# Growth factors as constants, opening loads and operand sums in another order, first batch's queries decayed by VectorE, in a fused retention and two-layer feed-forward kernel

## The chip, the cores and the metric

The kernel runs on one core of one Trainium2 chip. The metric is the device time of one execution in microseconds (us). Three runs of the kernel before took 589.05, 589.28 and 590.81 us; the median is 589.28 us.

## The reference

```python
# attention: q, k, v are (2 batches, 8 heads, 768, 64)
gamma = 1.0 - 2.0 ** (-5.0 - np.arange(H))
for t in range(S):
    state = gamma * state + outer(k[:, :, t], v[:, :, t])
    y[:, :, t] = scale * q[:, :, t] @ state
# x: 1536 tokens of 512
h = x @ w_in                      # 512 -> 2048
x = (h * sigmoid(1.702 * h)) @ w_out
xn = x / rms(x) * rms_g
x = (silu(xn @ w_gate) * (xn @ w_val)) @ w_out   # 512 -> 1536 -> 512
```

## The kernel before

Attention is done in 12 steps `a`: six chunks of 128 tokens for each of two batches, all eight heads in one step. A step has four kinds of products on TensorE: `scores` (L374, k by q, inside the chunk), `from_state` (L406, the decayed queries by the running state; the first chunk of a batch has none), `new_products` (L391, decayed k by v, summed in PSUM; the last chunk has none) and `from_chunk` (L419, masked scores by v). VectorE multiplies the scores by a mask (`masked`, L874) and scales the running sum into a state (`new_state`, L886 and L889). GpSimd multiplies k by a decay table (`decay_k`, L1008) and q by another (`decay_q`, L1016). ScalarE copies the result out (`copy_y`, L671). Steps go in pairs: scores of both, then the rest.

The running sum is never rescaled, so `decay_k` of chunk c needs a table that has grown by gamma to the power of -128 c. These tables are made at the start: two rows of the first table are loaded and broadcast by two small transfers, VectorE multiplies them, GpSimd takes the power -1 (L1037), VectorE refines it (L859 to L863) and multiplies tables 1 to 4 (L867, L870). Every step counts up the semaphore `decay_set`, and `masked(0)` and the first `decay_q` wait for its last value (GpSimd's wait stands after `decay_k(0)`).

Inputs come into four slots of 2048 columns, each in two transfers of 512 KB: q and k features first (`load`, semaphore `qk_in`), k and v tokens first (`load_kv`, `kv_in`). Two queues issue them, SyncE's and ScalarE's. In the trace SyncE issues, in this order, q/k of slots 0 and 1 (at 0.7 and 1.2 us), the mask (1.6), k/v of slot 2 (2.1), q/k of slots 2 and 3 (2.8 and 3.5), k/v of slot 3 (4.2) and the first weights (4.8); ScalarE issues the two rows (0.7 and 1.2), the decay table of 6 KB (1.6), k/v of slots 0 and 1 (2.1 and 2.9) and the query table (3.6). Later loads wait until a slot is free: `load(b)` for the scores and the decayed queries of step b - 4, `load_kv(b)` for its `y_done`.

The feed-forward layers use Strassen-like products: a hidden unit has seven products M1 to M7 of half-size blocks, each six matmuls of 384 columns (L457, L459, L460), from operands split into a high and a low part. Seven operands are made of x: B11, B21 and B22 are plain blocks of x; T1 to T4 are sums (`sum_x`, on VectorE; T1 and T3 together, then T2 from T3, then T4 from T2). ScalarE makes the high part (`split_x`, L599), VectorE the low (`lower_x`, L758); the weights go through `weight_sum` on GpSimd (four sums), `split_w` on ScalarE (L580) and `lower_w` on VectorE (L749). Semaphores count, so a product waits for the place of its operand in a fixed order: `UPPER` gives that of the high parts, and the low parts of the first phase go by the operand's own number. For the first phase this is woven into the attention steps of both engines by `if a == ...`; the rest comes at the start of the first hidden unit, n = 0. A hidden unit writes three PSUM banks. ScalarE copies M1 into the bank of M6 (`copy_m1`, L632), M5 into SBUF (`copy_m5`, L638), and the bank of M6 into SBUF (`copy_u2`, L644), which must be done before M7 adds to that bank.

All engines run their own program in order; nothing but the semaphores links them.

## Time and profile before

| | |
|---|---|
| median of three runs | 589.28 us (589.05 to 590.81) |
| the profiled execution's own time | 590.75 us |
| span of the profile | 588.96 us, shown as 589.0 |
| busy TensorE / VectorE / ScalarE / GpSimd | 576.1 / 354.0 / 298.2 / 175.7 us |
| DMA | 52.85 MB, mean 90 GB/s |

The profiled execution took 1.79 us more than its span, for what lies around it. A busy number counts the time in which an engine has an instruction in work; what limits the kernel is read from the idle stretches of TensorE and from its clock, which is granted at one of two levels, 1.2 GHz (0.50 in the windows view) or 2.4 GHz (1.00). The view has no record of the clock ahead of 10.17 us and shows 1.00 there; the matmuls' durations tell which level it was.

### The profile page before, as it was taken

To read this page: it belongs to the slowest core of one execution; us is meant where nothing else is said; L and a number is where in the kernel's file an instruction comes from. 1 tells how busy PE (TensorE), PEld (TensorE's weight loads), DVE (VectorE), ACT (ScalarE), POOL (GpSimd) and SP (SyncE) were. 2 spreads that over 40 slices of the span, in tenths; PEclk is the share of its full clock that TensorE was granted. 3 is DMA by queue.
4 is the path that set the end of the run, shared out by engine and by line. 5 is a ranking of instruction groups with operands and counts; after the bars stand their busy time and mean duration, and the time that the engine had idled before them with its cause. 6 is when DMAs were issued, how large, how long until landed. Compare 5 with 4: busy or idle time off the path is not lost.

```text
span 589.0 us, 9342 instructions
## 1 busy us (share of the span) xinstructions
PE 576.1 (98%) x3638; PEld 554.5 (94%) x3638; DVE 354.0 (60%) x459; ACT 298.2 (51%) x501; POOL 175.7 (30%) x189
## 2 busy tenths in 40 slices
PE   6899999999999999999999999999999999999997
PEld 6788999999999999999999999998889999998886
DVE  2379555566444665876435778668763666667332
ACT  1134666754334776645327655564534555554321
POOL 2758344100040544000223464420050545430000
PEclk9699999999999999999999999999999999999999
DMA  8892222322211222322112222223212422223202
GB/s 292 279 332 90 71 73 72 102 77 72 73 36 37 71 73 73 105 74 72 37 36 73 72 72 72 73 72 108 63 46 76 140 72 72 71 73 108 71 1 107
DMA packets 24652, 52.85 MB, mean 90 GB/s; under 512 B 2208, under 2 KB 2336, under 8 KB 24608
## 3 DMA queue, kind: packets, MB, share of 16 engines
q1 hardware_dynamic: 23744, 50.93, 28.4%
q10 hardware_dynamic: 864, 1.33, 0.6%
q8 instruction: 29, 0.48, 0.3%
q14 instruction: 15, 0.12, 0.1%
HBM read 49.10 MB, written 3.15 MB: 89 GB/s over the span
## 4 chain that ended last, share of the span: by engine, by line
PE 92%; issue 3%; DVE 2%; POOL 1%; DMA 1%; ACTq 0%; POOLq 0%; DVEq 0%
PE bank L507 20%; PE twin L507 20%; PE twin L457 11%; PE twin L460 10%; PE twin L459 10%; PE bank L460 6%; PE bank L457 6%; PE bank L459 6%; DMA arena<-tables 1%; PE bank L406 1%; PE bank L419 1%; PE bank L391 1%; PE twin L374 1%; DVE x_lo L758 1%; POOL arena L1016 1%
## 5 line engine op out<-in xcount | busy, mean ns | idle before, releaser
L749 DVE TENSOR_TENSOR w_lo<-raw,w_hi 128x512 fp32r<-128x512 f32 (+2 forms) x148 | 148.8, 1021 | 50.6 <-ACT w_hi L580 50.4
L1023 POOL TENSOR_TENSOR raw<-raw 128x256 f32<-128x256 f32 x40 | 30.6, 765 | 319.9 <-DMA raw<-w 319.9
L457 PE MATMUL twin<-x_hi,w_hi 128*128 128x384 f32 x360 | 120.6, 335 | 0.9 <-DVE w_lo L749 0.9
L460 PE MATMUL twin<-x_hi,w_lo 128*128 128x384 f32 x360 | 120.4, 334 | 0.0
L459 PE MATMUL twin<-x_lo,w_hi 128*128 128x384 f32 x360 | 120.3, 334 | 0.0
L580 ACT ACTIVATE w_hi<-raw 128x512 fp32r<-128x512 f32 (+2 forms) x148 | 109.0, 763 | 19.2 <-PE bank L507 7.6
L784 DVE TENSOR_TENSOR g_lo<-arena,g_hi 128x768 fp32r<-128x768 f32 x56 | 54.8, 979 | 75.9 <-ACT g_hi L610 75.9
L610 ACT ACTIVATE g_hi<-arena 128x768 fp32r<-128x768 f32 x56 | 47.5, 848 | 103.5 <-PE bank L507 103.5
L457 PEld LDWEIGHTS twin<-x_hi,w_hi 128*128 128x128 f32 x360 | 67.6, 188 | 1.2 <-DVE w_lo L749 1.2
L459 PEld LDWEIGHTS twin<-x_lo,w_hi 128*128 128x128 f32 x360 | 67.6, 188 | 0.0
L460 PEld LDWEIGHTS twin<-x_hi,w_lo 128*128 128x128 f32 x360 | 67.6, 188 | 0.0
L459 PE MATMUL bank<-x_lo,w_hi 128*128 128x384 f32 x200 | 66.9, 334 | 0.0
L457 PE MATMUL bank<-x_hi,w_hi 128*128 128x384 f32 x200 | 66.9, 334 | 0.0
L460 PE MATMUL bank<-x_hi,w_lo 128*128 128x384 f32 x200 | 66.9, 334 | 0.0
L1033 POOL TENSOR_TENSOR raw<-raw 128x256 f32<-128x256 f32 x40 | 45.1, 1128 | 0.0
L507 PE MATMUL twin<-g_lo,w_hi 128*128 128x384 f32 x128 | 42.8, 334 | 0.0
L507 PE MATMUL twin<-g_hi,w_lo 128*128 128x384 f32 x128 | 42.8, 334 | 0.0
L507 PE MATMUL bank<-g_hi,w_hi 128*128 128x384 f32 x128 | 42.8, 334 | 0.0
L507 PE MATMUL twin<-g_hi,w_hi 128*128 128x384 f32 x128 | 42.8, 334 | 0.0
L507 PE MATMUL bank<-g_hi,w_lo 128*128 128x384 f32 x128 | 42.8, 334 | 0.0
L507 PE MATMUL bank<-g_lo,w_hi 128*128 128x384 f32 x128 | 42.8, 334 | 0.0
L1029 POOL TENSOR_TENSOR raw<-raw 128x256 f32<-128x256 f32 x40 | 39.3, 981 | 3.1
(107 smaller groups left out, 1002.8 us busy)
## 6 DMA issues: line engine op xcount, KB each, us to landing
raw<-w SPq DMA_DIRECT2D x68, 512.0 KB, 3.7
arena<-attn_in SPq DMA_DIRECT2D x22, 512.0 KB, 6.5
out<-x SPq DMA_DIRECT2D x1, 1536.0 KB, 8.6
out<-x SPq DMA_DIRECT2D x6, 256.0 KB, 2.0
arena<-attn_in ACTq DMA_DIRECT2D x2, 512.0 KB, 10.7
arena<-tables SPq DMA_DIRECT2D x1, 512.0 KB, 7.5
arena<-tables ACTq DMA_DIRECT2D x1, 256.0 KB, 12.8
ident<-ident_in SPq DMA_DIRECT2D x1, 64.0 KB, 13.4
```

The source lines that it names most:

```text
L374: mm = pe.matmul(acc[2 * par + h][:, cols(p, P)], k[rows, cols(p, P)], q[rows, cols(p, P)], start=True, stop=True)
L457: pe.matmul(dst, w_hi[q][:, w], x_hi[:, x], start=start and kk == 0, stop=False, skip_group_check=True)
L459: pe.matmul(dst, w_hi[q][:, w], x_lo[:, x], start=False, stop=False, skip_group_check=True)
L460: mm = pe.matmul(dst, w_lo[q][:, w], x_hi[:, x], start=False, stop=kk == 1, skip_group_check=True)
L507: mm = pe.matmul(dst, a, x, start=f == 0 and k == 0, stop=f == TILES[layer] - 1 and k == 2, skip_group_check=True)
L580: act.activation(w_hi[q % 3][:, dst], src, ACT.Copy).then_inc(w_hi_done, 1)
L610: act.activation(g_hi[ft % 3][:, :], g32[:, cols(f, SEQ)], ACT.Copy).then_inc(g_hi_done, 1)
L749: dve.tensor_tensor(w_lo[q % 3][:, dst], src, w_hi[q % 3][:, dst].bitcast(F32), ALU.subtract)\
L784: dve.tensor_tensor(g_lo[ft % 3][:, :], g32[:, cols(f, SEQ)], g_hi[ft % 3][:, :].bitcast(F32), ALU.subtract).then_inc(g_lo_done, 1)
L1023: pool.tensor_tensor(s1, a21, a22, ALU.add).then_inc(w_sums, 1)
L1029: pool.tensor_tensor(s4, a12, s2, ALU.subtract).then_inc(w_sums, 1)
L1033: pool.tensor_tensor(a21, a11, a21, ALU.subtract).then_inc(w_sums, 1)
```

## The change

- The growth factors of chunks 1 to 4 are constants: 16 memsets of one column on VectorE and 16 on GpSimd, then one product of 32 columns on VectorE for all four tables. The two row loads, the power and its refinement are gone. `masked(0)` waits for `decay_set` 4, `decay_k(1)` for 1.
- Opening loads: q/k of slot 1 and k/v of slot 2 go to ScalarE's queue, k/v of slot 1 to SyncE's. ScalarE's order is decay table, k/v 0, q/k 1, query table, k/v 2; SyncE's is q/k 0, mask, k/v 1, q/k 2, q/k 3, k/v 3, weights.
- TensorE does `new_products(0)` between `scores(0)` and `scores(1)`.
- `decay_q` of steps 1 to 5 is VectorE's; GpSimd keeps steps 7 to 11. Each batch has its own semaphore.
- In the first phase the plain blocks are split first and T2, T3 and T4 later; in unit n = 0 T4 is summed and split after `copy_m5`, and the products come in the order M1, M5, M2, M3, M6, M7 instead of M1, M5, M6, M2, M3, M7. GpSimd waits for six low parts (`x_lo_done`) before the weight sums of the second unit.

```diff
-UPPER = {True: (B11, B21, T3, T1, B22, T2, T4), False: (B11, B21, T1, T2, B22, T3, T4)}
+UPPER = {True: (B11, B21, B22, T1, T3, T2, T4), False: (B11, B21, T1, T2, B22, T3, T4)}
+LOWER = {True: (B11, B21, T1, B22, T2, T3, T4), False: (B11, B21, T1, T2, B22, T3, T4)}
...
+        def growth(c, h):
+            return (1.0 - 2.0 ** (-5.0 - h)) ** (-CHUNK * c)
...
             load(0)
-            load(1)
             sp.dma_start(table[:, T_MASK:T_Q], tables[:, T_MASK:T_Q]).then_inc(mask_in, 16)
-            load_kv(2)
+            load_kv(1)
...
                 scores(a)
+                if a == 0:
+                    new_products(0)
                 scores(a + 1)
                 if a == 0:
-                    new_products(0)
                     from_state(0)
...
-            for k, row in enumerate((first_row, next_row)):
-
-                at_ = (CHUNK - 2) * k
-                act.dma_start(row, tables[at_:at_ + 1, T_K:T_K + HEADS].to_broadcast([P, HEADS])).then_inc(rows_in, 16)
             act.dma_start(table[:, 0:T_MASK], tables[:, 0:T_MASK]).then_inc(decay_in, 16)
-            for a in range(2):
-                act.dma_start(slot[a][:, 1024:2048], attn_in[BATCH * a, :, 1024:2048]).then_inc(kv_in[a], 16)
+            act.dma_start(slot[0][:, 1024:2048], attn_in[0, :, 1024:2048]).then_inc(kv_in[0], 16)
+            act.dma_start(slot[1][:, 0:1024], attn_in[BATCH, :, 0:1024]).then_inc(qk_in[1], 16)
             act.dma_start(table[:, T_Q:T_ALL], tables[:, T_Q:T_ALL]).then_inc(q_table_in, 16)
+            act.dma_start(slot[2][:, 1024:2048], attn_in[2 * BATCH, :, 1024:2048]).then_inc(kv_in[2], 16)
...
-            dve.wait_ge(rows_in, 32)
-            dve.tensor_tensor(growth, first_row, next_row, ALU.mult).then_inc(decay_set, 1)
...
+            for c in range(1, 3):
+                for h in range(HEADS):
+                    ins = dve.memset(factor(c, h), growth(c, h))
+            ins.then_inc(factors_set, 1)
+            dve.wait_ge(factors_set, 2)
             dve.wait_ge(decay_in, 16)
...
                 masked(a)
                 if a == 0:
                     new_state(0)
+                    decay_q(1)
                 masked(a + 1)
-                if a == 4:
+                if a < 4:
+                    decay_q(a + 2)
+                elif a == 4:
                     lower_x(0, B11)
...
                     if n > 0:
                         lower_w(r, 1)
                     else:
+                        sum_x(0, T4)
                         lower_x(0, T4)
...
+                    if n == 0:
+                        split_x(0, T4)
                     split_next(r, 0)
                     copy_u2(n)
...
                 if kind == "hidden":
+                    if r == 1:
+
+                        pool.wait_ge(x_lo_done, 6)
                     for k in range(4):
```

How the instructions move, at three places. First ScalarE's queue at the start of the program, before (L659 the rows, L660 the decay table, L662 k/v of slots 0 and 1, L663 the query table):

```order
L659 DMA arena<-tables 128x8 x2
L660 DMA arena<-tables 128x12
L662 DMA arena<-attn_in 128x1024 x2
L663 DMA arena<-tables 128x512
L665 ACT_TABLE_LOAD
```

and now (L673 the decay table, L674 k/v of slot 0, L675 q/k of slot 1, L676 the query table, L677 k/v of slot 2):

```order
L673 DMA arena<-tables 128x12
L674 DMA arena<-attn_in 128x1024
L675 DMA arena<-attn_in 128x1024
L676 DMA arena<-tables 128x512
L677 DMA arena<-attn_in 128x1024
```

The decay table and k/v of slot 0 stand first; the query table still has two loads of 512 KB ahead of it.

VectorE's first two pairs of steps, before (L874 `masked`, L886 and L889 `new_state`):

```order
L874 TENSOR_TENSOR arena<-twin,arena 128x1024 [waits scores_done,decay_set,mask_in]
L886 COPY arena<-bank 128x256 [waits kv_done]
L874 TENSOR_TENSOR arena<-twin,arena 128x1024 [waits scores_done]
L889 TENSOR_TENSOR arena<-bank,arena 128x256 [waits kv_done]
L889 TENSOR_TENSOR arena<-bank,arena 128x256 [waits cross_done,kv_done]
```

and now (L884 `masked`, L896 and L899 `new_state`, L910 `decay_q`):

```order
L884 TENSOR_TENSOR arena<-twin,arena 128x1024 [waits scores_done,decay_set,mask_in]
L896 COPY arena<-bank 128x256 [waits kv_done]
L910 TENSOR_TENSOR arena<-arena 128x512 [waits qk_in1,q_table_in]
L884 TENSOR_TENSOR arena<-twin,arena 128x1024 [waits scores_done]
L910 TENSOR_TENSOR arena<-arena 128x512 [waits qk_in2]
L899 TENSOR_TENSOR arena<-bank,arena 128x256 [waits kv_done]
L910 TENSOR_TENSOR arena<-arena 128x512 [waits cross_done,qk_in3]
L899 TENSOR_TENSOR arena<-bank,arena 128x256 [waits cross_done,kv_done]
```

The second mask now stands behind a `decay_q` that waits for the query table, and two more stand between the masks and the states.

ScalarE around the start of the first hidden unit, before (L599 `split_x`, L671 `copy_y`, L632 `copy_m1`, L638 `copy_m5`, L580 `split_w`, L644 `copy_u2`):

```order
L599 ACTIVATE x_hi<-x_0 128x768 [waits x_sums]
L671 ACTIVATE x_1<-bank 128x2x2x128 [waits y_done] x2
L599 ACTIVATE x_hi<-x_0 128x768 [waits x_sums]
L632 ACTIVATE twin<-twin 128x384 [waits probs_done,m1_done]
L638 ACTIVATE arena<-twin 128x384 [waits m5_done]
L580 ACTIVATE w_hi<-raw 128x768 [waits w_sums]
L644 ACTIVATE arena<-twin 128x384 [waits m6_done]
```

and now (L616, L685, L649, L655, L597, L661 in the same roles):

```order
L616 ACTIVATE x_hi<-x_0 128x768 [waits x_sums]
L685 ACTIVATE x_1<-bank 128x2x2x128 [waits y_done] x2
L649 ACTIVATE twin<-twin 128x384 [waits probs_done,m1_done]
L655 ACTIVATE arena<-twin 128x384 [waits m5_done]
L616 ACTIVATE x_hi<-x_0 128x768 [waits x_sums]
L597 ACTIVATE w_hi<-raw 128x768 [waits w_sums]
L661 ACTIVATE arena<-twin 128x384 [waits m6_done]
```

The split of T4, with its wait for VectorE's sum, has gone from ahead of `copy_m1` to between `copy_m5` and `copy_u2`.

## Rows read from the trace of the kernel before

**Rows 1.** Stretches: us, busy us (instructions) of each engine, TensorE clock, DMA share, GB/s.
```profile
13.59:23.83 10.24, 8.19 (x95) 7.34 (x92) 2.39 (x4) 1.19 (x2) 6.71 (x6) 0.50 0.91 330
23.83:57.00 33.17, 31.24 (x572) 28.89 (x570) 26.77 (x29) 11.43 (x18) 24.75 (x20) 1.00 0.65 223
77.00:575.00 498.00, 498.00 (x2764) 482.80 (x2763) 306.39 (x397) 268.97 (x452) 132.82 (x146) 1.00 0.25 71
```

**Rows 2.** Waits of TensorE over the whole span: us in total, times, longest.
```profile
PE bank L391 <- POOL arena L1008: 3.4, 2, 2.9
PE bank L406 <- POOL arena L1016: 2.8, 2, 2.0
```

**Rows 3.** Issues from 0.5, 1.5, 2.0 and 3.6 us on: count, KB, us to landing.
```profile
arena<-attn_in SPq DMA_DIRECT2D x1, 512.0 KB, 5.7
...
arena<-tables SPq DMA_DIRECT2D x1, 512.0 KB, 7.5
arena<-tables ACTq DMA_DIRECT2D x1, 6.0 KB, 7.7
...
arena<-attn_in SPq DMA_DIRECT2D x1, 512.0 KB, 9.6
arena<-attn_in ACTq DMA_DIRECT2D x1, 512.0 KB, 9.7
...
arena<-tables ACTq DMA_DIRECT2D x1, 256.0 KB, 12.8
```

**Rows 4.** Timeline, opening: start, us, engine, line, tiles, count [idle before <- releaser].
```profile
6.48 3.79 PE L374 MATMUL twin<-arena 64*128 64x128 f32 x32 [0.80 <-DMA arena<-attn_in]
...
12.01 1.04 POOL L1008 TENSOR_TENSOR arena<-arena 128x512 f32<-128x512 f32 x1 [2.12 <-DVE arena L870]
...
12.05 1.23 DVE L874 TENSOR_TENSOR arena<-twin,arena 128x1024 f32<-128x1024 f32 x1
...
13.76 1.98 PE L419 MATMUL bank<-arena 128*64 128x128 f32 x16
...
16.47 1.26 POOL L1016 TENSOR_TENSOR arena<-arena 128x512 f32<-128x512 f32 x1 [3.42 <-DMA arena<-tables]
...
17.79 1.97 PE L406 MATMUL bank<-arena 64*64 64x128 f32 x16 [2.05 <-POOL arena L1016]
...
19.69 1.12 PE L391 MATMUL bank<-arena 128*64 128x64 f32 x16
...
23.30 2.29 PE L374 MATMUL twin<-arena 64*128 64x128 f32 x32
```

**Rows 5.** Timeline, chunks 6 to 9, TensorE at its upper level.
```profile
37.20 2.06 PE L374 MATMUL twin<-arena 64*128 64x128 f32 x32
...
41.55 1.92 PE L419 MATMUL bank<-arena 128*64 128x128 f32 x32
...
45.84 1.97 PE L406 MATMUL bank<-arena 64*64 64x128 f32 x32
...
47.74 0.69 PE L391 MATMUL bank<-arena 128*64 128x64 f32 x16
```

**Rows 6.** Timeline, from attention to the first hidden unit, 58 to 61 us.
```profile
58.00 1.49 DVE L779 TENSOR_TENSOR x<-x 128x768 f32<-128x768 f32 x1
...
59.41 0.68 DVE L749 TENSOR_TENSOR w_lo<-raw,w_hi 128x512 fp32r<-128x512 f32 x1
...
59.52 0.84 ACT L599 ACTIVATE x_hi<-x 128x768 fp32r<-128x768 f32 x1 [1.42 <-DVE x L779]
...
60.27 0.47 ACT L632 ACTIVATE twin<-twin 128x384 f32<-128x384 f32 x1
...
60.84 0.41 PE L457 MATMUL twin<-x_hi,w_hi 128*128 128x384 f32 x1 [0.92 <-DVE w_lo L749]
```

**Rows 7.** Timeline, VectorE: one shape beside GpSimd's work and by itself.
```profile
35.45 1.80 DVE L749 TENSOR_TENSOR w_lo<-raw,w_hi 128x768 fp32r<-128x768 f32 x1
...
61.91 0.96 DVE L749 TENSOR_TENSOR w_lo<-raw,w_hi 128x768 fp32r<-128x768 f32 x1 [0.56 <-ACT w_hi L580]
```

More of the change, by code:

```diff
@@ L101, in transformer_kernel @@
         state = [part(256) for _ in range(2)]
-        k_table = [table[:, T_K:T_K + HEADS]] + [part(HEADS) for _ in range(1, CHUNKS - 1)]
+        factors = part((CHUNKS - 2) * HEADS)
+        later_k = part((CHUNKS - 2) * HEADS)
+        k_table = [table[:, T_K:T_K + HEADS]] + [later_k[:, HEADS * c:HEADS * c + HEADS] for c in range(CHUNKS - 2)]
         g_table = [None, table[:, T_G:T_G + PAIRS]] + [part(PAIRS) for _ in range(2, CHUNKS - 1)]
-        first_row, next_row = part(HEADS), part(HEADS)
-        growth, rest, power = part(HEADS), part(HEADS), part(HEADS)
-        minus_one = part(HEADS)
         used[0] = 0
@@ L134, in transformer_kernel @@
         probs_done = sem("probs_done")
-        q_decayed = sem("q_decayed")
+        q_decayed = [sem(f"q_decayed{i}") for i in range(BATCH)]
         k_decayed = sem("k_decayed")
@@ L481, in hidden @@
                     fourth(n - 1)
-                pe.wait_ge(w_lo_done, lo_at[r] + 2)
-                pe.wait_ge(m1_copied, n + 1)
-                product(6, n, 2, 1, 2, T2, False)
-                product(2, n, 0, 0, 2, B21, False)
-                pe.wait_ge(m5_copied, n + 1)
-                product(3, n, 1, 1, 3, B22, False)
+                if n > 0:
+                    pe.wait_ge(w_lo_done, lo_at[r] + 2)
+                    pe.wait_ge(m1_copied, n + 1)
+                    product(6, n, 2, 1, 2, T2, False)
+                    product(2, n, 0, 0, 2, B21, False)
+                    pe.wait_ge(m5_copied, n + 1)
+                    product(3, n, 1, 1, 3, B22, False)
+                else:
+                    pe.wait_ge(m1_copied, n + 1)
+                    product(2, n, 0, 0, 2, B21, False)
+                    pe.wait_ge(w_lo_done, lo_at[r] + 2)
+                    pe.wait_ge(m5_copied, n + 1)
+                    product(3, n, 1, 1, 3, B22, False)
+                    product(6, n, 2, 1, 2, T2, False)
                 pe.wait_ge(u2_copied, n + 1)
@@ L890, in new_state, with decay_q @@
                 ins.then_inc(state_done, 1)
+            def decay_q(a):
+                r, x = a % SLOTS, cross_at(a)
+                if a == 1:
+                    dve.wait_ge(q_table_in, 16)
+                dve.wait_ge(qk_in[r], 16 * (a // SLOTS) + 16)
+                if x >= 2:
+                    dve.wait_ge(cross_done, x - 1)
+                dve.tensor_tensor(q_dec[x % 2], slot[r][:, 0:512], table[:, T_Q:T_Q + 512], ALU.mult)\
+                   .then_inc(q_decayed[0], 1)
             dve.wait_ge(mask_in, 16)
-            dve.wait_ge(decay_set, 2 * CHUNKS - 1)
+            dve.wait_ge(decay_set, CHUNKS - 2)
             for a in range(0, STEPS, 2):
@@ L998, in _ @@
         def _(pool):
-            pool.memset(minus_one, -1.0).then_inc(one_set, 1)
+            for c in range(3, CHUNKS - 1):
+                for h in range(HEADS):
+                    ins = pool.memset(factor(c, h), growth(c, h))
+            ins.then_inc(factors_set, 1)
             pool.memset(minus_half[:, :], -0.5).then_inc(half_set, 1)
```

60 lines of the change are left out of this document (25 added, 35 removed).

## The prediction

> **What bounds the kernel now.** I read the stretches first, then TensorE's waits, then the transfers and the timeline of the stretches that are not full. From 77 to 575 us TensorE is busy for 498.00 of 498.00 us at its upper clock level [rows 1]: nothing that the change touches lies there, and what it gains or loses ahead of it moves all of it as a block. So the reader needs the first 60 us alone. Between 23.8 and 57 us TensorE is busy for 31.24 of 33.17 us at 2.4 GHz [rows 1]; two steps take 2.06 (scores), 1.97 (`from_state`), twice 0.69 (`new_products`) and 1.92 us (`from_chunk`), 7.3 in all [rows 5], so attention too is bound by TensorE once it runs. The time that can be had stands before: from 13.59 to 23.83 us the granted clock is 0.50, the level of 1.2 GHz [rows 1], and TensorE waits for GpSimd twice, at most 2.9 us for the decayed keys and 2.0 us for the decayed queries [rows 2].
>
> **The opening before.** Scores 0 and 1 run from 6.48 to 10.27 us, at the lower level by their duration (3.79 us for what takes 2.06 later) [rows 4, 5]. `decay_k(0)` starts at 12.01 [rows 4], which the view puts down to VectorE's table, but GpSimd waits there only for the decay table and for k/v of slot 0, and the latter, issued at 2.1, needs 9.7 us and lands at 11.8 [rows 3]. The first mask starts at 12.05, held by the tables. `from_state(1)` starts at 17.79, behind `decay_q` at 16.47, which waited for the query table [rows 4]: issued at 3.6, 12.8 us to landing [rows 3]. Scores 2 and 3 start at 23.30 [rows 4]. That is the mark I count against: from there on the order of TensorE's work is the same.
>
> **The loads now.** Bytes stay (8 KB less), so the last opening load lands as before. Before, q/k of slot 0 landed at 6.4, q/k 1 and the mask each 1.3 us after the one ahead (mask 1.6 + 7.5 = 9.1), while ScalarE's small transfers went beside them one to one, the decay table landing at 1.6 + 7.7 = 9.3; then k/v 0 and k/v 2 came down side by side in 2.6 us, to 11.7 and 11.8 [rows 3]. By this pattern now: decay table beside q/k 0, both by 6.6; k/v 0 beside the mask, both by 9.1; k/v 1 beside q/k 1, 11.7; the query table beside q/k 2, 1.9 us more, 13.6 (before 16.4 [rows 3]); k/v 2 beside q/k 3, 16.2. The Trainium skill (DMA: Bandwidth & Descriptors, section "Issuing engines are not separate DMA queues") says that transfers of several engines interleave on the same DMA engines and that a second issuer saves only issue time; by that rule alone the new split would be worth nothing. It is right on the bytes, and this part rests on their order alone.
>
> **The tables.** The 16 memsets of VectorE and 16 of GpSimd lie before 6.6 us, where both engines have nothing else; no row has VectorE's one-column memset, its price is between nothing and the small products of this trace, 0.2 us each, 3.2 us from 1.3 on: over by 4.5, hidden. The tables are ready about 7.5, ahead of the mask's 9.1, so their cost is zero either way.
>
> **TensorE's opening, step by step.** Durations at the lower level: scores of one step 1.9, `from_chunk` 1.98, `from_state` 1.97, `new_products` 1.12 [rows 4].
> 1. scores(0) 6.48 to 8.4. `decay_k(0)` 9.1 to 10.2 (1.04 [rows 4]). `new_products(0)` 10.3 to 11.4.
> 2. scores(1) from the landing of q/k 1, 11.7, to 13.6. Mask 0 is done at 9.2 + 1.23 = 10.4, so `from_chunk(0)` follows to 15.5.
> 3. `decay_q(1)` starts on VectorE at 13.6. No row has it there; the nearest is a product of the same 128x512 size by itself, 0.68 us [rows 6], and the upper end is 0.68 x 1.80 / 0.96 = 1.3 us beside GpSimd's work [rows 7]. I take 0.7: GpSimd has only `decay_k` left. Done at 14.3 (14.9), mask 1 at 15.5 (16.1); `from_state(1)` starts at 15.5 at either price.
> 4. Clock. It rose at 10.17, TensorE having run without a break since 6.48, and at 23.83, having run since 17.79 with no gap worth a row. Here TensorE runs without a break from 11.7: by the two cases the rise comes at 15.4 to 17.7, and I take 16.5. Then `from_state(1)` ends at 17.0, `new_products(1)` (0.69 [rows 5]; k/v 1 landed at 11.7) at 17.7, `from_chunk(1)` (0.96) at 18.6, `new_products(2)` at 19.3; its decayed keys are there at 16.2 + 1.04 to 1.3 = 17.5.
> Scores 2 and 3 start at 19.3 instead of 23.3: **4.0 us gained**, 4.6 with the rise at 15.4, 3.4 with it at 17.7.
>
> **Does it last to 57 us?** The next loads hang on the scores and `y_done` of steps 0 to 3, which come earlier as well. q/k 4 is in hand at about 20, q/k 5 by 21.7, against a need at 26. VectorE per pair: two masks 2.46, two states 0.84, two `decay_q` 1.4 to 2.6, at most 5.9 of the 7 us that TensorE takes; it is no bound. The queue of VectorE is what to watch: a mask behind a `decay_q`, whose wait for `cross_done` is one step back and over by then. I cost this at zero: GpSimd's waits for loads in this stretch (1.9 us of TensorE idle [rows 1]) stay, since load and use move together. If it is no zero, it is a rival below.
>
> **The handover.** Before, after M1 and M5, TensorE waits 0.92 us, until 60.84. The view names `lower_w`, but that is `w_lo` at 59.41 + 0.68 = 60.1; `copy_m1` ends at 60.27 + 0.47 = 60.74, late because ScalarE first split T4 (to 60.36) behind VectorE's sum (to 59.49) [rows 6]. From 60.84 M6, M2 and M3 run, six matmuls at about 0.173 us each, 1.04 a product, so M7 starts at 63.95. Now, in the same time frame, M1 to M6 run through from 57.5 for five products, to 62.7; the T2 part is lowered about 57.8 and T3 about 58.8 (masks over at 55, sum, two lowerings at 0.95, ScalarE's 0.84 between). M7 then waits for `copy_u2`, no longer covered by M2 and M3: ScalarE has the T4 split until 61.3, the next unit's weights until 62.2, then `copy_u2` from 62.9 to 63.4 after M6's last write. M7 at 63.5: **0.5 us gained**, between 0 (ScalarE 0.5 late) and 0.9 (no wait). GpSimd's new wait ends with T3 at 58.8; its first sum serves the weights split at 61.3, so 1.2 to 2 us of slack lie in that chain.
>
> **Sum.** 590.75 - 4.0 - 0.5 = **586.2 us**, against the profiled execution, which stood 1.5 us above the median of 589.28. I do not carry this 1.5 over whole: the runs shown stand at 589.1 to 589.3 and at 590.8, which a clock that rises at another moment of the opening would give, and the new opening has its own rise, already bounded.
>
> **Rivals.**
> - *More than the forecast.* The clock is up for most of the opening, as the faster runs shown suggest. For it: 1.5 us between equal programs. 586.2 - 1.2 = 585.0.
> - *The clock rises late.* The new opening has breaks before 11.7 (8.4 to 10.3, 11.4 to 11.7); should one load come later than drawn, the unbroken run starts later. With the lower level kept to 23.8, scores 2 and 3 start at 21.4 and end at 24.6, not 25.6: 1.0 + 0.5 gained, 589.2; with a rise at 20.4, 588.1. I take 588.6.
> - *The loads do not follow.* From 23.8 to 57 us the DMA engines show 0.65 busy for 223 GB/s only [rows 1]. If what slows them is not demand, slots fill no earlier and TensorE gives the 4.0 back as waits: 590.2. Against it: k/v 3 and the first weights land early enough and the stretch has 1.9 us of idle in all.
> - *VectorE and GpSimd hinder each other at the handover* (slower). A 128x768 product took 1.80 us beside GpSimd's work and 0.96 alone [rows 7]. If all six VectorE operations from the sum of T2 to the lowering of T4 and the weights behind them ran at the worse price, 0.84 to 1.08 more each, 7 us in all, less 1.2 of slack, M7 and the second unit would come 6 us late: 592.4. It decides once T3's low part is over 5.6 us late. Against it: GpSimd's second unit now waits for that part and it has only `decay_q` 11 behind it. The Trainium skill (GPSIMD Engine Reference, section "Key points") states that GpSimd shares its SBUF interfaces with VectorE, contending with its instructions of two SBUF inputs, which all these and the moved `decay_q` are; by that rule the move of five queries buys nothing for free.
> - *The change does what it says for the tables only*: were k/v 0 still last of its group, at 11.8, the decayed keys would come as before; this is a part of the late-clock case.
>
> **Chances.** Forecast 0.62, more 0.13, late clock 0.12, loads 0.08, hindrance 0.05. A measurement of this kernel tells about 0.3%, 1.8 us: below 587.5 is faster, above 591.0 slower. Faster 0.62 + 0.13 = 0.75; same 0.12 + 0.08 = 0.20; slower 0.05. The range goes from 584.7, the better case with the clock's 0.3 beyond, to 588.6, the late clock's middle; outside lie the loads and the hindrance and a half of the late clock, about 0.2.
>
> **What would show it.** Right: `decay_k(0)` starts near 9.1, the first mask near 9.2, `decay_q(1)` near 13.6 on VectorE; scores 2 at 19 to 20; the clock's long low stretch ends before 18; `copy_m1` follows M1 by 0.1 and a wait of 0.7 to 0.9 stands before M7. Wrong: k/v 0 or the query table landing as late as before, a low clock beyond 20 us, waits of TensorE for `decay_q` or masks in steps 2 to 5, or for low parts after 58 us.

## The result, and the profile after

| | before | changed |
|---|---|---|
| median (lowest to highest) | 589.64 us (589.05 to 590.81) | 584.75 us (584.47 to 585.02) |
| profiled execution, its span | 590.75, 588.96 us | 584.9, 583.1 us |
| busy TensorE / VectorE / ScalarE / GpSimd | 576.1 / 354.0 / 298.2 / 175.7 us | 573.5 / 358.5 / 298.3 / 171.6 us |

The changed kernel takes 0.9915 of the time, interval 0.9897 to 0.9932: 4.9 us less. The forecast was 586.2, which is 3.1 under the median it had before it. So the sign was right and the gain was larger than forecast. Against the profiled execution, on which the sum was made, the changed one gains 5.9 where 4.5 was summed; that execution of the kernel before, at 590.75, stood 1.1 above the median of 589.64, so the marks read from it below make each gain look up to 1 us larger than the medians do.

The windows view of the changed kernel; its columns are those of [rows 1]. The first two lines are the opening and the rest of attention, the last three lines answer to [rows 1], the last of them ending at 569 because everything is 6 us earlier:

```profile
6.00:24.00 18.00, 15.03 (x234) 13.60 (x232) 10.60 (x16) 1.58 (x3) 5.84 (x6) 0.81 1.03 406
24.00:36.00 12.00, 10.82 (x205) 10.06 (x202) 9.91 (x9) 5.56 (x9) 8.71 (x8) 1.00 0.93 310
...
13.59:23.83 10.24, 10.24 (x180) 9.38 (x178) 7.64 (x10) 1.41 (x3) 3.59 (x4) 0.90 1.03 399
23.83:57.00 33.17, 31.64 (x507) 29.32 (x503) 29.11 (x29) 14.56 (x23) 22.41 (x18) 1.00 0.60 202
77.00:569.00 492.00, 492.00 (x2729) 476.80 (x2728) 302.12 (x392) 265.12 (x443) 129.86 (x142) 1.00 0.25 71
```

From 77 us on TensorE is full as before, so again all that was won was won ahead of it. In 13.59 to 23.83 TensorE has no idle time left, and its mean clock is 0.90, not 0.50: a fifth of 10.24 us at the lower level, so the clock rises at about 15.6. New to me was the first line: from 6 to 24 us the DMA engines are full (share 1.03) and move 406 GB/s (before: 0.96 and 362), and from 24 to 36 they are still 0.93 busy (before: 0.79).

TensorE's waits of 0.2 us and more in the changed kernel (us in total, times, longest), against [rows 2]:

```profile
PE bank L397 <- POOL arena L1036: 2.8, 1, 2.8
PE bank L413 <- POOL arena L1044: 1.2, 1, 1.2
PE bank L434 <- DVE ones L864: 1.1, 1, 1.1
PE twin L465 <- ACT arena L661: 0.6, 1, 0.6
PE bank L397 <- issue: 0.3, 1, 0.3
PE bank L482 <- DVE w_lo L764: 0.2, 1, 0.2
PE twin L380 <- DMA arena<-attn_in: 0.2, 1, 0.2
```

The wait for the first decayed keys (L397) is as long as before, but it ends 3.7 us earlier (9.52 instead of 13.20). That for the first decayed queries is gone. The wait for GpSimd's `decay_q(7)` (L413 <- L1044) was there before, as the second of the two in the L406 row of [rows 2], and has grown from 0.75 to 1.2. The two at the handover are new: 0.6 before M7, which the prediction drew as 0.7 to 0.9, and 0.2 for the low part of the weights.

The issues view of the changed kernel, issues from 0.7 us, from 1.2 (mask and k/v 0), from 1.7 (k/v 1 on SyncE's queue) and from 2.1 on (query table, then k/v 2, which is issued at 3.0), against [rows 3]:

```profile
arena<-attn_in SPq DMA_DIRECT2D x1, 512.0 KB, 4.6
arena<-tables ACTq DMA_DIRECT2D x1, 6.0 KB, 4.8
...
arena<-tables SPq DMA_DIRECT2D x1, 512.0 KB, 6.7
arena<-attn_in ACTq DMA_DIRECT2D x1, 512.0 KB, 7.0
...
arena<-attn_in SPq DMA_DIRECT2D x1, 512.0 KB, 8.8
...
arena<-tables ACTq DMA_DIRECT2D x1, 256.0 KB, 10.6
...
arena<-attn_in ACTq DMA_DIRECT2D x1, 512.0 KB, 12.6
```

Issue plus this time gives the landing: decay table 5.5 (drawn as 6.6), mask 7.9 (9.1), k/v 0 at 8.2 (9.1), k/v 1 at 10.5 (11.7), query table 12.7 (13.6), k/v 2 at 15.6 (16.2). The order is the one drawn; all of it is 0.6 to 1.2 us early.

The timeline of the changed kernel, opening, against [rows 4]:

```profile
7.88 1.22 DVE L884 TENSOR_TENSOR arena<-twin,arena 128x1024 f32<-128x1024 f32 x1 [1.46 <-DMA arena<-tables]
8.33 1.04 POOL L1036 TENSOR_TENSOR arena<-arena 128x512 f32<-128x512 f32 x1 [6.97 <-DMA arena<-attn_in]
...
10.80 2.08 PE L380 MATMUL twin<-arena 64*128 64x128 f32 x16 [0.16 <-DMA arena<-attn_in]
12.72 0.69 DVE L910 TENSOR_TENSOR arena<-arena 128x512 f32<-128x512 f32 x1 [1.62 <-DMA arena<-tables]
12.81 1.97 PE L426 MATMUL bank<-arena 128*64 128x128 f32 x16
...
14.71 1.53 PE L413 MATMUL bank<-arena 64*64 64x128 f32 x16
...
16.17 0.69 PE L397 MATMUL bank<-arena 128*64 128x64 f32 x16
...
18.12 2.06 PE L380 MATMUL twin<-arena 64*128 64x128 f32 x32
```

Each step waits for its load: the mask, the keys, the second scores and the queries all name a DMA as their releaser. `decay_q(1)` takes 0.69 on VectorE, as taken. Scores 2 and 3 start at 18.12, before at 23.30, drawn for 19.3.

The handover in the changed kernel (timeline, 51 to 60 us), against [rows 6, 7]:

```profile
51.35 0.44 PE L482 MATMUL twin<-x_hi,w_hi 128*128 128x384 f32 x1
...
53.48 1.12 POOL L1051 TENSOR_TENSOR raw<-raw 128x256 f32<-128x256 f32 x1 [5.15 <-DVE x_lo L773]
...
53.92 1.50 DVE L794 TENSOR_TENSOR x<-x 128x768 f32<-128x768 f32 x1
...
56.33 1.32 DVE L773 TENSOR_TENSOR x_lo<-x,x_hi 128x768 fp32r<-128x768 f32 x1 [0.92 <-ACT x_hi L616]
...
57.58 1.48 DVE L764 TENSOR_TENSOR w_lo<-raw,w_hi 128x768 fp32r<-128x768 f32 x1
...
57.58 0.44 PE L465 MATMUL twin<-x_hi,w_hi 128*128 128x384 f32 x1 [0.58 <-ACT arena L661]
...
59.11 0.44 PE L482 MATMUL bank<-x_hi,w_hi 128*128 128x384 f32 x1 [0.22 <-DVE w_lo L764]
```

GpSimd was held for 5.15 us by its new wait, until VectorE had lowered T3. Its weight sums then fall beside VectorE's last operand work, which takes 1.32 to 1.50 us where 0.96 would do [rows 7]. Up to M7 the handover is shorter than before, 6.23 us from the start of M1 (51.35 to 57.58) instead of 6.66 (57.39 to 64.05); from M7 to the second matmul of the second unit it is longer, 1.81 us instead of 1.21.

To place the gain I use four marks of TensorE: scores 2, scores 10 (the last pair), the first matmul of M1 in the first unit, and the second matmul of the second unit (its first is drawn out by the wait in front of it in one kernel and not in the other).

```
kernel                     scores 2  scores 10     M1   2nd unit
before                        23.30      51.46  57.39      65.26
changed                       18.12      45.43  51.35      59.39
difference                    -5.18      -6.03  -6.04      -5.87
```

The last difference is that of the spans (5.86).

### The profile page after: what moved, and what is told of

Read it like the earlier page. It is cut to its first block, busy times and chain, and to the rows that moved or that the text cites. A ratio compares the mean times of both kernels' runs of the same rounds, so it can differ in the third digit from the quotient of the medians.

```text
span 583.1 us, 9363 instructions
## 1 busy us (share of the span) xinstructions
PE 573.5 (98%) x3638; PEld 551.9 (95%) x3638; DVE 358.5 (61%) x473; ACT 298.3 (51%) x501; POOL 171.6 (29%) x198
## 4 chain that ended last, share of the span: by engine, by line
PE 90%; DVE 3%; DMA 3%; issue 1%; POOL 1%; ACT 0%; ACTq 0%; POOLq 0%; DVEq 0%
PE bank L524 20%; PE twin L524 20%; PE twin L465 10%; PE twin L468 10%; PE twin L467 10%; PE bank L465 6%; PE bank L468 6%; PE bank L467 6%; DMA arena<-attn_in 3%; DVE x_lo L773 1%; DVE arena L884 1%; DVE w_lo L764 1%; PE bank L565 0%; PE twin L380 0%; DVE t L786 0%
## 5 line engine op out<-in xcount | busy, mean ns | idle before, releaser
L1051 POOL TENSOR_TENSOR raw<-raw 128x256 f32<-128x256 f32 x40 | 32.6, 814 | 317.7 <-DMA raw<-w 312.6
L597 ACT ACTIVATE w_hi<-raw 128x512 fp32r<-128x512 f32 (+2 forms) x148 | 109.0, 763 | 18.0 <-PE bank L524 7.6
L1061 POOL TENSOR_TENSOR raw<-raw 128x256 f32<-128x256 f32 x40 | 46.8, 1170 | 0.0
L1057 POOL TENSOR_TENSOR raw<-raw 128x256 f32<-128x256 f32 x40 | 39.3, 984 | 3.1
## 6 DMA issues: line engine op xcount, KB each, us to landing
ident<-ident_in SPq DMA_DIRECT2D x1, 64.0 KB, 12.8
```

The lines of the kernel that those rows point to most:

```text
L597: act.activation(w_hi[q % 3][:, dst], src, ACT.Copy).then_inc(w_hi_done, 1)
L1051: pool.tensor_tensor(s1, a21, a22, ALU.add).then_inc(w_sums, 1)
L1057: pool.tensor_tensor(s4, a12, s2, ALU.subtract).then_inc(w_sums, 1)
L1061: pool.tensor_tensor(a21, a11, a21, ALU.subtract).then_inc(w_sums, 1)
```

## The experiments

Each was timed beside runs of the kernel before (medians 589.5 to 589.9 in the four sets, 11 to 17 runs each), and I compare medians with 584.75 of the changed kernel, which was timed in a set of its own (before 589.64). Its four runs lie within 0.6 us, so a difference of 0.3 us or less says nothing.

**Which part pays.** The kernel before with the constant tables alone, the load order kept:

```diff
-            for k, row in enumerate((first_row, next_row)):
-                at_ = (CHUNK - 2) * k
-                act.dma_start(row, tables[at_:at_ + 1, T_K:T_K + HEADS].to_broadcast([P, HEADS])).then_inc(rows_in, 16)
...
+            for c in range(1, 3):
+                for h in range(HEADS):
+                    ins = dve.memset(factor(c, h), growth(c, h))
```

> The kernel before with nothing but the constant tables: the two broadcasts, the power and its refinement are gone; loads, products and operand order are those of before. The run with the broadcasts put back cost 4.1 us. If the broadcasts and not VectorE's chain were what held the opening, this part alone brings most of the whole change: k/v 0 lands near 9 us, the query table near 13.5, and the kernel takes 586.0 to 587.3 us. If the gain needs the new order of the loads and VectorE's queries beside it, as my sum had it (my drawing moved k/v 0 from 11.8 to 9.1 by the order): 587.8 to 589.0 us.

Measured: 586.75 us (586.19 to 587.61), 0.9947 of before, 0.9935 to 0.9959: 3.1 us gained, three fifths of the whole, from a part that the prediction priced at zero. The issues view of this kernel, issues from 0.7, 1.2 and 2.1 us on:

```profile
arena<-tables ACTq DMA_DIRECT2D x1, 6.0 KB, 4.2
...
arena<-attn_in ACTq DMA_DIRECT2D x1, 512.0 KB, 7.6
...
arena<-tables ACTq DMA_DIRECT2D x1, 256.0 KB, 11.2
```

The decay table lands at 4.9, k/v 0 at 1.2 + 7.6 = 8.8 and the query table at 2.1 + 11.2 = 13.3. Before, they landed at 9.3, 11.8 and 16.4 [rows 3]. In the same order of loads all that stood behind the rows comes 3 us and more earlier. Only 8 KB were taken away. The chain that computed the factors on VectorE and GpSimd is gone in this kernel too; the next one has the rows without the chain.

The reverse: the changed kernel, with the two row loads put back at the head of ScalarE's queue; nothing computes with them.

```diff
+            for k, row in enumerate((first_row, next_row)):
+                at_ = (CHUNK - 2) * k
+                act.dma_start(row, tables[at_:at_ + 1, T_K:T_K + HEADS].to_broadcast([P, HEADS])).then_inc(rows_in, 16)
             act.dma_start(table[:, 0:T_MASK], tables[:, 0:T_MASK]).then_inc(decay_in, 16)
```

> The changed kernel with the two broadcast row loads put back ahead of the decay table on ScalarE's queue; nothing reads them but a wait on ScalarE that ends early. In the changed kernel q/k of slot 0 landed at 5.5 us instead of 6.4 and every opening load some 0.8 to 1.0 us earlier than I had drawn. Theory A (the 256 small packets of the broadcasts cost DMA time ahead of everything): q/k 0 lands at 6.3 to 6.5 again, k/v 0 and q/k 1 are 1 to 2 us later, and the kernel takes 585.9 to 587.0 us. Theory B (the start of the transfers varies from run to run, or it is the reordering): landings within 0.3 us of the changed kernel's, time 584.5 to 585.2 us.

Measured: 588.87 us (587.42 to 590.27), 0.9985, 0.9974 to 0.9996: 4.1 us lost, nearly all of the gain. So without the chain, with the new order and all the rest, the changed kernel is only 0.8 better than the one before as long as the rows stand at the head. Its issues view (from 1.5 and 2.0 us on), where the second row, the decay table and k/v 0 are:

```profile
arena<-attn_in SPq DMA_DIRECT2D x1, 512.0 KB, 8.5
arena<-tables ACTq DMA_DIRECT2D x1, 4.0 KB, 7.3
arena<-tables ACTq DMA_DIRECT2D x1, 6.0 KB, 8.6
...
arena<-attn_in ACTq DMA_DIRECT2D x1, 512.0 KB, 10.7
```

The second row lands at 1.2 + 7.3 = 8.5, 0.8 after the mask, the 6 KB of the decay table at 1.7 + 8.6 = 10.3 beside SyncE's k/v 1 (1.7 + 8.5), and k/v 0 at 12.8. Each transfer on ScalarE's queue, of 4 KB or of 512, took about the time of one of 512 KB on SyncE's. The two queues' packets from 5.0 to 5.6 us (packets, MB, busy share; q1 has SyncE's loads, q10 ScalarE's) show how:

```profile
q1 hardware_dynamic: 56, 0.20, 82.3%
q10 hardware_dynamic: 52, 0.00, 4.5%
```

Packet for packet the queues take turns, and a row, cut into one piece of 32 bytes for each of 128 partitions, needs as many turns as a load of 512 KB in pieces of 4 KB. In the changed kernel the same stretch has 36 and 32 packets, of 0.12 MB each. The start suffers as well: from 2 to 4 us the DMA engines move 154 GB/s here and 140 in the kernel before, against 228 in the changed one. TensorE shows it as one wait:

```profile
PE bank L399 <- POOL arena L1042: 7.2, 1, 7.2
```

It is 4.4 us longer than in the changed kernel. The same two loads at the end of ScalarE's queue, behind k/v 2:

```diff
             act.dma_start(slot[2][:, 1024:2048], attn_in[2 * BATCH, :, 1024:2048]).then_inc(kv_in[2], 16)
+            for k, row in enumerate((first_row, next_row)):
+                at_ = (CHUNK - 2) * k
+                act.dma_start(row, tables[at_:at_ + 1, T_K:T_K + HEADS].to_broadcast([P, HEADS])).then_inc(rows_in, 16)
```

> The changed kernel with the two broadcast loads put back, but at the end of ScalarE's queue, behind k/v of slot 2; nothing reads them. If they cost 4.1 us by standing ahead of k/v 0, each small packet taking a turn of the ring like a large one: 584.6 to 585.3 us here, at most 0.5 us over the changed kernel, k/v 0 landing near 8.3. If 256 small packets cost DMA time as such, wherever they stand: 586.5 us or more.

Measured: 585.63 us (585.21 to 587.14), 0.9935, 0.9923 to 0.9947: 0.9 lost. Here k/v 0 lands at 1.2 + 7.3 = 8.5, 0.3 later than in the changed kernel, and only what is under way at the end of the queue (k/v 3, the first weights) comes about 1.5 us later. So the rows cost by their place: 4.1 us at the head, 0.9 at the end. The turns are taken either way, from other loads.

The changed kernel with the old order and split of the loads, without the rows:

```diff
             load(0)
+            load(1)
             sp.dma_start(table[:, T_MASK:T_Q], tables[:, T_MASK:T_Q]).then_inc(mask_in, 16)
-            load_kv(1)
+            load_kv(2)
...
-            act.dma_start(slot[1][:, 0:1024], attn_in[BATCH, :, 0:1024]).then_inc(qk_in[1], 16)
+            act.dma_start(slot[1][:, 1024:2048], attn_in[BATCH, :, 1024:2048]).then_inc(kv_in[1], 16)
```

> The changed kernel with the opening loads in the order of the kernel before, the broadcasts still gone. If the order carries the gain (my step on the loads): k/v 0 lands near 10.2 and the query table near 15.3 instead of 12.8, from_state(1) starts near 16.8 instead of 14.7, and the kernel takes 586.0 to 587.5 us. If the order is worth nothing because the transfers share the same engines and only the bytes and small packets count: 584.5 to 585.2 us.

Measured: 585.63 us (585.06 to 586.24), 0.9933, 0.9919 to 0.9947: the new order is worth 0.9. It does not even show at the first mark: scores 2 start at 17.52, 0.6 earlier than in the changed kernel. TensorE then waits 0.8 us for the decayed keys of the next pair, and scores 4 start at 25.23, 0.4 later.

GpSimd decays all the queries again, the rest as changed:

```diff
-                if a < 4:
-                    decay_q(a + 2)
-                elif a == 4:
+                if a == 4:
...
-                    if b > CHUNKS:
+                    if b % CHUNKS > 0:
                         decay_q(b)
```

> The changed kernel with the queries of all steps decayed by GpSimd again, behind the query table as before. If VectorE's part matters: GpSimd does decay_q(1) at 12.7 to 14.0, then decay_k(1), decay_k(2) and the queries 2 and 3 one after the other, new_products(1) waits until about 15.2 and the second pair for its queries; 585.3 to 586.5 us. Rival (it only frees an engine that was no bound once the query table comes early): 584.6 to 585.2 us. A gain, under 584.3 us, would mean that VectorE with queries was the later engine in the second half of attention.

Measured: 584.94 us (584.64 to 585.11), 0.992, 0.9906 to 0.9935: 0.2 more, no difference that these runs can tell.

The old places of the plain parts and sums, the old order of products and no wait of GpSimd, the rest as changed:

```diff
-UPPER = {True: (B11, B21, B22, T1, T3, T2, T4), False: (B11, B21, T1, T2, B22, T3, T4)}
+UPPER = {True: (B11, B21, T3, T1, B22, T2, T4), False: (B11, B21, T1, T2, B22, T3, T4)}
...
+            split_x(0, T4)
...
-                        pool.wait_ge(x_lo_done, 6)
```

> The changed kernel with the operand order, the products' order in the first unit and the T4 sum and split of the kernel before, and without GpSimd's wait for six low parts. My forecast had 0.5 us for this part: then 585.2 us. What the two traces show is that the handover from the last attention product to the second unit's first takes 7.76 us in the changed kernel and 7.52 before: then this kernel takes 584.3 to 584.8 us, no slower than the changed one. Rival (the new order pays inside attention, where the changed kernel gained another 0.9 us after step 2): 585.5 to 585.9 us.

Measured: 585.93 us (585.53 to 586.47), 0.9939, 0.9925 to 0.9953: this part is worth 1.2, but not at the handover. Its waits of TensorE:

```profile
PE bank L397 <- issue: 1.0, 2, 0.6
PE twin L465 <- DVE w_lo L763: 0.8, 1, 0.8
PE bank L426 <- DVE arena L883: 0.3, 1, 0.3
```

From M1 to the second unit it takes 52.36 to 60.16, 7.80 us, less than the changed kernel's 8.04. What it loses lies ahead of M1, inside attention. VectorE is late with a mask by 0.3 us (L426), behind parts that it lowers there. `new_products` starts late twice; the longer wait, 0.6 at 38.52, stands behind a `decay_k` of GpSimd that waited for its load until 36.75 and then took 1.67 us beside a sum of VectorE, where the changed kernel's ran at 35.31 and took 1.04. So the 1.2 is not shown to be the masks' alone. The four parts (3.1 for tables and rows, added to the kernel before; 0.9, 0.2 and 1.2, taken out of the changed one) add up to 5.4, against 4.9 measured: they overlap little.

**Whether the clock pays.** The prediction placed the clock's rise in the sum and made a clock that is up early the first rival. The kernel before, with eleven products of ones behind the first scores, that fill TensorE's wait and whose result nothing reads:

```diff
                 if a == 0:
+                    for _ in range(11):
+                        pe.matmul(gate[1][:, 0:P], ones[:, :], ones[:, :], start=True, stop=True)
                     new_products(0)
```

> The kernel before with 11 more 128x128 products of ones after the first two steps' scores, into a bank that nobody has in use, so that TensorE has no idle stretch between 10.3 and 13.2 us; they compute nothing that is kept. If the low clock from 13.6 to 23.8 us was what its last stretch of the opening waited for (my step 4 and the rival of the early clock): the clock is up from 10.2 on in the profile and the kernel takes 587.3 to 588.6 us, with less spread between runs than 588.4 to 591.1. If the loads bind there anyway: 589.3 to 590.0 us with the clock up all the same.

Measured: 589.71 us (588.28 to 591.48), 0.9993, 0.9982 to 1.0004. The clock of 6 to 24 us went from 0.72 to 0.91, that is from 10.1 to 3.2 us at the lower level, and the median stayed. TensorE's waits in it:

```profile
PE bank L406 <- POOL arena L1018: 4.3, 2, 3.0
PE bank L391 <- POOL arena L1010: 1.6, 1, 1.6
```

They were 2.8 and 3.4 before [rows 2], and the filler itself takes the place of a part of the second. The faster TensorE reached the decayed queries earlier and waited for them: `from_state(1)` starts at 17.80, as before (17.79). But what is left of the lower level now lies right behind that wait (the clock is 0.57 from 17.8 to 21.8 us), in the work that leads to scores 2. They start at 22.36, 0.9 earlier than in the profiled execution before.

The median hides more than it shows here. Sorted by the mean granted clock that each run lists, the runs of the kernel before (56, the four sets together) and of the one with the filler have these mean times:

```
mean clock   before                   with the filler
0.991        590.05 (39 runs)         -
0.994        589.60 (10)              591.08 (2)
0.996        589.20 (3)               -
0.997        588.56 (4)               589.85 (6)
0.999, 1.0   -                        588.47 (4)
```

In both kernels the runs with the higher clock are the shorter ones, by about 1.5 us and more. At the same mean clock of 0.997 the kernel with the filler is 1.3 us slower, so the filler has a price of its own, or leaves the lower level where it hurts more, and the equal medians do not say that the clock is worth nothing. Nor is it shown which way the cause runs: a run that waits longer for a load can lose the clock by it, as in the kernel with the rows back, where it falls at 11.1 us, inside the wait of 7.2. The gain of the whole change is not the clock's: at 0.993 and 0.994 three runs of the changed kernel have a mean of 584.80, 4.8 under the ten of the kernel before. Of the 4.1 us that the rows cost at the head, 3.3 are left at that clock (588.12, five runs, against 584.80), and of the 3.1 of the tables alone 2.1 to 2.5 at mean clocks of 0.994 to 0.997 (five runs); the rest may have come by way of the clock. The same filler in the changed kernel, with ten products:

```diff
+                    for _ in range(10):
+                        pe.matmul(gate[1][:, 0:P], ones[:, :], ones[:, :], start=True, stop=True)
```

> The changed kernel with 10 more products of ones between the scores of step 0 and new_products(0), to hold the clock up. In the runs so far the clock rose at 15.7, 15.0, 13.7 and 13.8 us without a gain in step with it, since new_products(4) then waits for k/v of slot 0, which lands at 22.3 to 23.4 at a DMA rate of about 400 GB/s. If the loads are the bound of the changed opening: 584.3 to 584.9 us, no gain over 0.4 us. If the clock still is: 583.2 to 584.0 us.

Measured: 584.71 us (584.53 to 585.6), 0.9915, 0.9902 to 0.9927. The clock of 6 to 24 us is 1.00, all four runs have a mean of 0.999 or 1.0, and nothing is won. Where the lower level was, this wait stands in the profiled execution, the slowest of the four:

```profile
PE bank L397 <- issue: 3.2, 2, 1.7
```

The one of 1.7 us ends 0.1 us after GpSimd's `decay_k` of step 2 and stands behind k/v 2, the load that it reads: `decay_k` at 16.94 had waited 5.34 us for it. In the changed kernel k/v 2 had landed at 15.6, so part of this wait may be the spread of that load between executions.

**What bounds attention now.** Three kernels take away, one by one and together, what the changed kernel's trace offered. First, `decay_q(7)` goes ahead of GpSimd's weight sums, since TensorE waits 1.2 us for it:

```diff
-                    if b > CHUNKS:
+                    if b > CHUNKS + 1:
                         decay_q(b)
...
+                if a == 4:
+                    decay_q(7)
```

> The changed kernel with decay_q(7) ahead of GpSimd's two weight sums of the third pair. In its profile from_state(7) waits 1.2 us for this query product, which stands behind the two sums. If that wait is what it seems: 583.4 to 583.9 us. If the step after it waits as much longer (k/v for new_products(8), landing at 35.5): 584.4 to 584.9 us.

Measured: 585.03 us (584.5 to 585.7), 0.9918, 0.9905 to 0.9931. The wait of 1.2 is gone, and waits of 1.9 us in all for `new_products` (L397, longest 0.8) have come. Then the first weights and two constants, which do not belong to attention, behind the loads of the next slots:

```diff
-            load_weights(0)
...
+                if a == 4:
+                    load_weights(0)
```

> The changed kernel with the first weights issued behind k/v of step 5 and the identity and the gain behind the second weights, so that 0.58 MB at about 400 GB/s, 1.4 us, leaves the way of the loads that the second to fourth steps wait for. If bytes in the opening are now the bound: k/v for step 4 lands near 21 instead of 22.3 to 23.4 us, no wait for new_products(4), and the kernel takes 583.3 to 584.2 us. If the next waits take its place (GpSimd's weight sums and the loads of steps 8 and 9): 584.4 to 584.9 us.

Measured: 584.97 us (584.58 to 585.37), 0.9921, 0.9908 to 0.9934: no gain. GpSimd had k/v 4 at 20.75, 1.6 us earlier than in the changed kernel, but the next k/v load that it waits for at 29.90, 1.65 later, and the last no earlier. And all three, filler, `decay_q(7)` and late weights, in one kernel:

```diff
+                    for _ in range(10):
+                        pe.matmul(gate[1][:, 0:P], ones[:, :], ones[:, :], start=True, stop=True)
...
+                if a == 4:
+                    load_weights(0)
...
+                if a == 4:
+                    decay_q(7)
```

> The weights late, decay_q(7) ahead of the weight sums, and the 10 products of ones that hold the clock up, in one. Each of the last two gave nothing by itself with the loads as the bound. If the loads' bound is what hid them: 582.0 to 583.3 us, better than the weights late alone by 0.7 or more. If the attention stretch is bound by other things (the loads of the later steps): within 0.4 us of the weights late alone.

Measured: 584.79 us (583.93 to 586.95), 0.9924, 0.9907 to 0.9941: no gain. Its stretches (columns as in [rows 1]):

```profile
6.00:24.00 18.00, 15.95 (x276) 14.42 (x272) 10.90 (x17) 2.06 (x4) 5.21 (x5) 1.00 1.03 401
24.00:36.00 12.00, 10.90 (x200) 10.10 (x197) 10.64 (x11) 5.19 (x8) 7.91 (x7) 1.00 0.95 331
```

and its waits:

```profile
PE bank L398 <- issue: 2.4, 4, 0.8
PE twin L381 <- DMA arena<-attn_in: 1.3, 2, 0.7
```

Full clock, no wait for `decay_q(7)`, and yet 2.05 of 18 us and 1.10 of 12 us idle, with TensorE now waiting for q/k loads by name. M1 starts at 51.48, in the changed kernel at 51.35. Three different remedies gave the same time, and the DMA engines are 0.91 to 1.03 busy from 6 to 36 us in all three. Two of the six runs of this last kernel, those with a mean clock of 0.997, took 586.67 and 586.95 us, the other four 583.93 to 585.02, so a gain of a few tenths would not show. I read this as a stage that goes at the pace of its loads. It is read, not shown: no kernel with fewer bytes was tried.

Last, the changed kernel without GpSimd's new wait:

```diff
-                    if r == 1:
-
-                        pool.wait_ge(x_lo_done, 6)
```

> The changed kernel without GpSimd's wait for six low parts ahead of the weight sums of the second unit. My slower rival had the two engines hinder each other at the handover; in the changed kernel's profile the sums do run beside VectorE's last operand work all the same (the T4 sum 1.50 instead of 0.95 us, the T4 low part 1.32, the second unit's weights 1.48 instead of 0.96) and the second unit starts 0.2 us late for them. If the wait protects more than it delays: 584.9 to 585.6 us, T2's and T3's low parts at 1.3 us and more instead of 0.96. If the wait only makes the sums meet the later operations: 584.1 to 584.7 us, the second unit starting without a wait for VectorE.

Measured: 584.15 us (583.2 to 585.69), 0.9909, 0.9892 to 0.9925. The lowest median of all the kernels, 0.6 below the changed one, but the ranges overlap and the gain is not established. Its timeline at the handover shows what the wait does:

```profile
48.80 1.35 POOL L1057 TENSOR_TENSOR raw<-raw 128x256 f32<-128x256 f32 x1
...
53.05 0.94 DVE L794 TENSOR_TENSOR x<-x 128x768 f32<-128x768 f32 x1
...
54.91 0.96 DVE L773 TENSOR_TENSOR x_lo<-x,x_hi 128x768 fp32r<-128x768 f32 x1 [0.91 <-ACT x_hi L616]
...
55.78 0.95 DVE L764 TENSOR_TENSOR w_lo<-raw,w_hi 128x768 fp32r<-128x768 f32 x1
```

GpSimd's sums are done by 51 us, and the three operations of VectorE take 0.94 to 0.96 instead of 1.32 to 1.50. From M1 (50.35) to the second unit it is 7.56 us, against 8.04 with the wait, 7.80 with the old order and no wait, 7.87 before. By these single executions the new order of products is worth 0.2 to 0.3 us, and the wait that came with it costs 0.5. M1 itself starts 1.0 us earlier than in the changed kernel, ahead of anything that the wait touches, so the difference of the spans is not the wait's alone.

The marks of the kernels that carry the argument:

```
kernel                     scores 2  scores 10     M1   2nd unit   median
before                        23.30      51.46  57.39      65.26   589.64
tables alone                  20.23      47.25  54.36      62.15   586.75
changed                       18.12      45.43  51.35      59.39   584.75
rows back at the head         21.64      48.92  54.84      62.88   588.87
old load order                17.52      45.60  51.53      59.57   585.63
old places of the parts       17.56      45.85  52.36      60.16   585.93
without GpSimd's wait         17.69      44.58  50.35      57.91   584.15
all three remedies            17.37      45.71  51.48      59.08   584.79
```

Scores 2 come as early as 17.37 and the median does not follow: in all the kernels with scores 2 before 18 us but the one without GpSimd's wait, the time that the first pairs win over the changed kernel is given back before scores 10.

## Why the prediction was right or wrong

*"What bounds the kernel now."* Right: the first 60 us alone decided.

*"The loads now."* This is the step that failed. It counted the two row loads as 8 KB, said "the last opening load lands as before", and got the gain of k/v 0 and of the query table out of their new order. The runs show that each of them, in 128 packets of 32 bytes, held ScalarE's queue for about as long as a 512 KB load, and with them gone all behind them moves up by 3 us or more, even in the old order. The pattern was even in the text, which had the small transfers go beside SyncE's "one to one". It was used to place the decay table and not to price the two turns that the change removes. Tables and rows alone are worth 3.1 us, the order 0.9; the prediction had it as 0 and 4.0. So its last rival, that the change "does what it says for the tables only", given no gain of its own, was the larger part of the result.

The Trainium skill (DMA: Bandwidth & Descriptors, section "Issuing engines are not separate DMA queues") was set against the new split. On bytes it holds, and the small worth of the split, 0.9 us, speaks for it too. What paid here is another thing: on one queue, the rows that stood first held up what stood behind them, however few bytes they had.

*"TensorE's opening."* Right in each link, and the sum of 4.0 was short by 1.2. Loads landed about 0.9 earlier than drawn, of which 0.8 reaches scores(1) (12.81 to their end instead of 13.6); the last three steps before scores 2 took 1.95 (16.17 to 18.12), not 2.3, since such steps overlap by more than I drew. Scores(0) ran at the upper level (1.16 us, not 1.9), but nothing waited for them. The clock rose at 15.6, not 16.5, but that is in `from_state(1)`, about 1 us from its start, as drawn. The landing of q/k 0 at 5.3 against 6.4 before is in part the rows (5.7 with them back, 4.8 with the tables alone); the rest of its spread I can't explain.

*The clock as the measure of more or less.* The first rival's time, 585.0, was near the result, but by another mechanism: at like mean clock the change gains 4.8 us. What it rests on, that equal programs differ with their clock, is borne out by the kernel before, 590.05 at 0.991 and 588.56 at 0.997. In the changed kernel the full clock won nothing. What the late clock would have cost stays open, since no run kept the changed kernel at the lower level.

*"Does it last to 57 us? I cost this at zero."* It lasted, and 0.86 us were added: from scores 2 to M1 it takes 33.23 us, before 34.09. With the old places of the parts it takes 34.80. So this is where the plain operands first pay, 1.2 by the medians. How much of it is the late mask and how much GpSimd's late and slow `decay_k` is not separated. The prediction looked for that part's worth at the handover alone.

*"The handover: 0.5 gained."* Wrong in sign, by the trace: 7.87 before, 8.04 after. `copy_m1` and the wait before M7 came as drawn, and M7 itself 0.4 earlier, for 0.5 drawn. The loss of 0.6 lies behind M7, which the sum left out. Not drawn there was what the rival of hindrance names: GpSimd's sums beside VectorE's operand work. It was priced at 6 us (its own terms, six operations at 0.84 to 1.08 less 1.2 of slack, give 3.8 to 5.3) and came to 0.5, because T3's low part was in time, as that rival's counter-argument had it.

*The loads do not follow.* The rival at 590.2 did not come, but its idea may be what limits the kernel now: the DMA engines are full to 24 us and nearly so to 36.

*The sum:* 4.0 became 5.2, 0 became 0.86, 0.5 became -0.2; together 5.9 on the profiled executions instead of 4.5. The runs of before in the later sets have medians of 589.5 to 589.9, so the caution with the 1.5 us between the profiled execution and the first median was in place, but the three runs shown were on the low side. By the medians the change gains 4.9, near the 4.5 summed, by luck: the rows' 3.1 was in no term, and the order, which was to carry the 4.0, is worth 0.9.

## What to carry to other kernels

Price a small transfer at the head of a queue by the landing times of what stands behind it, not by its bytes: take it away, or put it last, before reordering the large ones. A low clock beside a wait may cost nothing where the work that it slows would wait later anyway, as in the changed kernel. A filler tests this, but it has a price of its own and moves the lower level elsewhere, so sort the runs by their clock before reading the median. And when an edit adds a wait that moves work of another engine, look whom that work now runs beside.

## What the runs showed of the hardware that I had not expected

- A row of 4 KB, broadcast to 128 partitions in 32-byte pieces, delayed what stood behind it on its queue by about as much as a transfer of 512 KB on the other queue took, as the two queues' packets alternated (56 and 52 of them from 5.0 to 5.6 us, with 0.20 and 0.00 MB): with two rows at the head k/v 0 landed at 12.8, without them at 8.2, and 4.1 us of the kernel's time went with it.
- Sixteen memsets of one column take VectorE 0.27 us together and GpSimd 0.59; the prediction had allowed up to 3.2 us for VectorE's. They are the lines at 1.38 and 0.73 of the changed kernel's timeline:

```profile
0.73 0.59 POOL L1026 MEMSET arena<- 128x1 f32 x16 [0.29 <-POOLq L1141]
...
1.38 0.27 DVE L871 MEMSET arena<- 128x1 f32 x16
```

- VectorE's 128x768 operations took 1.32 to 1.50 us beside GpSimd's sums, and 0.94 to 0.96 in the kernel in which those sums had moved away, with all else as it was. This agrees with the Trainium skill (GPSIMD Engine Reference, section "Key points"), by which the two engines share SBUF interfaces; the traces put it at 1.4 to 1.6 times here.
